# A retention and mixture-of-experts kernel: the retention cut into twelve steps of 64 tokens of both batches, its products in 64 by 64 tiles

## The reference

```python
for t in range(S):                       # retention, per batch and head
    state = gamma[h] * state + outer(k[t], v[t])
    y[t] = q[t] @ state / sqrt(D)        # x = y, heads side by side, 512 wide
logits = x @ w_gate                      # 8 experts
local_gate = sigmoid(x @ w_local)
for each batch, for s in range(S):       # routing: a scan along the tokens
    e = argmax(logits[s]) if s == 0 or local_gate[s] < 0.5 else e_of_token_before
    p = softmax(logits[s])
    out[s] = p[e] * (relu(x[s] @ w1[e]) @ w2[e])
```

## Time and profile before

| | us |
|---|---|
| median of 3 runs | 266.32 (265.81 to 267.69) |
| the profiled execution | 265.87 |
| its span in the trace | 264.1 |
| TensorE's granted clock over the span | 0.993 of full |
| retention loop, first masked product to `x_transpose` | 8.52 to 66.61 |
| first product of the experts (L1085) | 68.74 |

### The profile page before, as it was taken

One profiled execution on the slowest core, in us unless ns is written; L12 is line 12 of the kernel. 1 busy time (PEld: TensorE's weight loads), 2 busy tenths in 40 slices (PEclk: granted clock), 3 DMA queues, 4 the chain that ended last, 5 costly groups with the idle time before them and its releaser, 6 DMA issues.

```text
span 264.1 us, 4970 instructions
## 1 busy us (share of the span) xinstructions
PE 253.7 (96%) x1935; PEld 216.3 (82%) x1935; DVE 196.4 (74%) x408; ACT 135.5 (51%) x253; POOL 60.1 (23%) x57
## 2 busy tenths in 40 slices
PE   8899999998999999999999999999999999999991
PEld 3688887887887888888988888898898889889891
DVE  2445899996996796987789598588859858877700
ACT  1313637457559273485477438457644835753310
POOL 0473333531004331006104201500510240011011
PEclk9999999999999999999999999999999999999997
DMA  5999999942202818187538808925861890620000
GB/s 183 359 414 412 413 412 412 426 182 79 82 1 72 367 64 315 70 318 249 211 130 306 353 2 318 351 96 196 313 273 37 315 380 33 251 104 34 0 37 34
DMA packets 11386, 56.82 MB, mean 215 GB/s; under 512 B 1751, under 2 KB 2135, under 8 KB 9570
## 3 DMA queue, kind: packets, MB, share of 16 engines
q1 hardware_dynamic: 7056, 45.95, 45.2%
q0 software_dynamic: 2560, 7.34, 7.3%
q10 hardware_dynamic: 1746, 3.19, 3.2%
HBM read 50.19 MB, written 7.34 MB: 218 GB/s over the span
## 4 chain that ended last, share of the span: by engine, by line
PE 80%; DVE 12%; ACT 2%; DMA 2%; issue 2%; POOLq 0%; SPq 0%; DVEq 0%
PE ps L1085 21%; PE ps L1087 10%; PE ps L1104 10%; PE ps L1105 10%; PE ps L1106 10%; PE ps L972 3%; PE ps L984 3%; PE ps L1065 2%; DVE scores_masked L754 2%; DVE w_split L767 2%; PE ps L1017 2%; PE ps L1007 2%; PE ps L1128 2%; ACT slot_values L487 2%; DMA qkv_sb<-qkv 2%
## 5 line engine op out<-in xcount | busy, mean ns | idle before, releaser
L1085 PE MATMUL ps<-x_sorted_T,w_split 128*128 128x480 f32 (+1 forms) x288 | 89.4, 370 | 0.2 <-DVE x_sorted_T L780 0.2
L1087 PE MATMUL ps<-x_sorted_T,w_split 128*128 128x240 f32 (+1 forms) x288 | 75.5, 262 | 0.0
L774 DVE TENSOR_TENSOR w_split<-w_raw,w_split 128x1024 fp32r<-128x1024 f32 x56 | 66.1, 1219 | 6.8 <-ACT w_split L493 6.8
L787 DVE TENSOR_REDUCE h_sums<-ps 128x240 f32<-128x480 f32 (+1 forms) x72 | 43.0, 598 | 23.8 <-PE ps L1087 22.8
L1085 PEld LDWEIGHTS ps<-x_sorted_T,w_split 128*128 128x128 f32 x288 | 54.1, 188 | 7.1 <-issue 0.3
L493 ACT CAST w_split<-w_raw 128x1024 fp32r<-128x1024 f32 x56 | 55.8, 1042 | 4.7 <-DMA w_raw<-w 4.7
L1087 PEld LDWEIGHTS ps<-x_sorted_T,w_split 128*128 128x128 f32 x288 | 54.7, 190 | 0.3
L502 ACT ACTIVATE hT<-h_sums 128x240 fp32r<-128x240 f32 (+1 forms) x72 | 27.1, 380 | 52.8 <-DVE h_sums L787 52.8
L1104 PE MATMUL ps<-w_split,hT 128*128 128x512 f32 x120 | 48.3, 402 | 0.0
L386 POOL DMA_INDIRECT out<-y_rows,scatter_idx x16 | 17.1, 1068 | 135.0 <-ACT y_rows L510 130.7
L1105 PE MATMUL ps<-w_split,hT 128*128 128x512 f32 x120 | 47.4, 395 | 0.0
(11 more groups left out here) (130 smaller groups left out, 265.6 us busy)
## 6 DMA issues: line engine op xcount, KB each, us to landing
w_raw<-w SPq DMA_DIRECT2D x14, 2048.0 KB, 9.2
qkv_sb<-qkv SPq DMA_DIRECT2D x22, 512.0 KB, 12.9
w_raw<-w SPq DMA_DIRECT2D x8, 512.0 KB, 15.5
x_rows<-x_rows_sb ACTq DMA_DIRECT2D x12, 256.0 KB, 6.7
qkv_sb<-qkv SPq DMA_DIRECT2D x2, 256.0 KB, 13.2
out<-y_rows,scatter_idx POOLq DMA_INDIRECT x16, 5.0
x_gathered<-x_rows,gather_idx POOLq DMA_INDIRECT x15, 7.8
c_route_sb<-c_route SPq DMA_DIRECT2D x1, 146.0 KB, 9.5
```

Of the source, the lines that this page charges most:

```text
L774: V.tensor_tensor(ws[:, par, 1, half, at:at + PIECE], raw[:, half, at:at + PIECE], ws[:, par, 0, half, at:at + PIECE].bitcast(fp32), ALU.s ...
L787: V.tensor_reduce(hs[:, f % 3, 0:n * ROWS], h_ps[f % 3][:, 0:2 * n * ROWS].rearrange("p (a t) -> p t a", a=2), AX.X, ALU.add).then_inc(h_s ...
L1085: MM(at[:, 0:2 * w].rearrange("p (a t) -> p a t", a=2), ws[:, par, 0, 0, cols], xTs[:, k, :, sub], start=(k == 0), stop=(k == KD - 1), ski ...
L1087: last = MM(at[:, w:2 * w], ws[:, par, 1, 0, cols], xTs[:, k, 0, sub], start=False, stop=(k == KD - 1), skip_group_check=True)
```

## The change

The retention's step is 64 tokens (C = 64) of both batches side by side, 12 steps again. The scores of a step are then 64 by 64 blocks, one for each head and batch, and all four phases have 16 float32 products of 64 by 64 tiles with 64 streamed, in an order in which four that follow each other use four different quarters of the array. PE's phases sum: `from_state` and `state_products` now miss at one step each (the first and the last) instead of at two.

With it:

- masks and `q_decays` are for 64 tokens. `masked` is one instruction of 512 elements a partition, not two.
- the state is kept in SBUF for both batches (512 elements a partition, not 256) and DVE adds a step's products to it (`st + u_ps`). Its decay goes into q: POOL makes `q_now` (`q_scale`, 256 elements a partition, once a step) and multiplies q by it.
- the step's output has one PSUM buffer of two banks, and `from_state` waits for ACT's copy of the step before. `from_chunk` is in two halves around `state_products`.
- the order on PE, ACT and DVE inside a step is new; the routing groups have 2, 3, 3 and 4 steps. A group's scan is two instructions (one for each batch), `to_col` has two products for each step.
- the pieces of expert 0's weights are loaded at other steps, the last three behind all of q, k, v; the router's and w1's rows are reordered on the host to fit the new order of heads.

```diff
+C = S // 12
-NX = NC * B
+NX = S // C
-GC = 3
-GROUPS = NX // GC
+GROUP_AT = (0, 2, 5, 8, NX)
```

The loads on SP:

```diff
+            e0_piece(0)
             for m in range(4, NX):
                 if m >= SLOTS:
                     sp.wait_ge(y_done, m - SLOTS + 1)
                 load_half(m, 0)
                 load_half(m, 1)
-                if m >= 4:
-                    e0_piece(m - 4)
+                if m in (5, 6, 7, 9):
+                    e0_piece({5: 1, 6: 2, 7: 3, 9: 4}[m])
+            for p in range(5, 2 * PIECES):
+                e0_piece(p)
```

POOL:

```diff
+            def q_scale(m):
+                pool.wait_ge(qdec_ready, 1)
+                if m > 1:
+                    pool.wait_ge(q_ready, m - 1)
+                nc.gpsimd.tensor_tensor(q_now[:, :, :], q_dec[:, :, :],
+                                        s_dec[:, m, :].unsqueeze(2).to_broadcast([P, HP, C]),
+                                        ALU.mult).then_inc(q_scaled, 1)
+            for m in range(NX - 1):
+                if m == 0:
+                    k_decayed(0)
+                    q_scale(1)
+                else:
+                    q_scale(m + 1)
+                    k_decayed(m)
+                q_decayed(m + 1)
```

ACT's loop:

```diff
             for m in range(NX):
+                xT_out(m)
+                if m in KEEP_AT:
+                    exps(KEEP_AT[m])
+                    keep_row(KEEP_AT[m])
+                if m in E0_MID:
+                    e0_high(E0_MID[m])
+                if m == GROUP_AT[2] + 3:
+                    slot_values(1, range(2))
+                if m < NX - 1:
+                    logits_out(m)
+                    rows_out(m)
+                if m == GROUP_AT[1] + 3:
+                    slot_values(0, range(size(0)))
+                if m == GROUP_AT[2] + 3:
+                    slot_values(1, range(2, size(1)))
+                for p in E0_END.get(m, ()):
+                    e0_high(p)
```

DVE, its two operations of a step and its loop:

```diff
             def masked(m):
                 dve.wait_ge(qk_done, m + 1)
-                for r in range(2):
-                    V.tensor_tensor(sm[:, m % 2, r, :, :], sc_ps[r], masks[:, r, :, :], ALU.mult).then_inc(m_ready, 1)
+                V.tensor_tensor(sm[:, m % 2, :, :, :].rearrange("p r n t -> p r (n t)"), sc_ps,
+                                masks.rearrange("p r n t -> p r (n t)"), ALU.mult).then_inc(m_ready, 1)
             def state(m):
-                dve.wait_ge(u_done, b * (NC - 1) + c + 1)
-                V.tensor_tensor(st[:, :, :], u_ps, s_dec[:, c + 1, :].unsqueeze(2).to_broadcast([P, HP, D]),
-                                ALU.mult).then_inc(s_ready, 1)
+                dve.wait_ge(u_done, m + 1)
+                dve.wait_ge(qk_done, m + 2)
...
+                    V.tensor_tensor(st[:, :, :, :], st[:, :, :, :], u_ps, ALU.add).then_inc(s_ready, 1)
...
             for m in range(NX):
+                if m in COL_AT:
+                    route_c(COL_AT[m])
+                if m < NX - 1:
+                    state(m)
+                    masked(m + 1)
+                if m in COL_AT:
+                    route_d(COL_AT[m])
+                    if COL_AT[m] < 2:
+                        slot_match(COL_AT[m])
...
+                if m in A_AT:
+                    route_a(A_AT[m])
+                if m in KEEP_AT:
+                    route_b(KEEP_AT[m])
+                if m in E0_LOW:
+                    e0_low(E0_LOW[m])
```

PE, `qk` (the other phases in the same manner) and its loop:

```diff
+                for n in range(HP):
+                    for r in range(2):
+                        for b in range(B):
+                            rows, half = slice(r * D, (r + 1) * D), slice(b * C, (b + 1) * C)
+                            last = MM(sc_ps[half, r, n * C:(n + 1) * C], io[rows, s, 1, n, half],
+                                      io[rows, s, 0, n, half], start=True, stop=True)
...
             for m in range(NX):
+                if m in COL_AT:
+                    to_col(COL_AT[m])
+                if m > 0:
+                    from_state(m)
+                from_chunk(m, 0)
+                if m < NX - 1:
+                    state_products(m)
+                from_chunk(m, 1)
+                if m == NX - 1:
+                    break
+                qk(m + 1)
+                if m in KEEP_AT:
+                    to_rows(KEEP_AT[m])
...
+                rows_and_logits(m)
```

The tables of steps:

```diff
+A_AT = {GROUP_AT[g + 1]: g for g in range(GROUPS - 1)}
+KEEP_AT = {at + 1: g for at, g in A_AT.items()}
+COL_AT = {at + 2: g for at, g in A_AT.items()}
+E0_MID = {6: 2}
+E0_END = {2: (0,), 4: (1,), 7: (3,), 9: (4,), 10: (5, 6)}
+E0_LOW = {3: 0, 5: 1, 6: 2, 8: 3, 9: 4, 10: 5, 11: 6}
```

More of the change, by code:

```diff
@@ L987, in state_products @@
-            def state_products(m):
-                b, c = divmod(m, NC)
-                s = m % SLOTS
-                pe.wait_ge(k_ready, b * (NC - 1) + c + 1)
-                for n in range(HP):
-                    for r in range(2):
-                        rows = slice(r * D, (r + 1) * D)
-                        last = MM(u_ps[rows, n, :], kd[:, m % 2, 2 * n + r, :], io[:, s, 3, n, rows],
-                                  start=(c == 0 and n == 0), stop=True, skip_group_check=True)
-                last.then_inc(u_done, 1)
@@ L999, in from_chunk @@
-            def from_chunk(m):
-                s = m % SLOTS
-                pe.wait_ge(kv_in[s], 16 * (m // SLOTS + 1))
-                pe.wait_ge(m_ready, m * 2 + 2)
-                for n in range(HP):
-                    for r in range(2):
-                        rows = slice(r * D, (r + 1) * D)
-                        last = MM(y_ps[m // (NX - 1)][rows, n, :], io[:, s, 3, n, rows], sm[:, m % 2, r, n, :],
-                                  start=(m % NC == 0 and n == 0), stop=True, skip_group_check=True)
-                last.then_inc(y_done, 1)
+                pe.wait_ge(q_ready, m)
@@ new lines, in from_state @@
+                pe.wait_ge(s_ready, m)
+                pe.wait_ge(xT_ready, m)
+                for pair in range(2):
+                    for b in range(B):
+                        for r in range(2):
+                            for n in range(2 * pair, 2 * pair + 2):
+                                rows = slice(r * D, (r + 1) * D)
+                                MM(y_at(n, r, b), st[rows, b, n, :], qd[rows, m % 2, n, b * C:(b + 1) * C],
+                                   start=(pair + b == 0), stop=False, skip_group_check=True)
@@ new lines, in from_chunk @@
+            def from_chunk(m, other):
+                s = m % SLOTS
+                if other == 0:
+                    pe.wait_ge(kv_in[s], 16 * (m // SLOTS + 1))
+                    pe.wait_ge(m_ready, m + 1)
+                else:
+                    pe.wait_ge(y_half, m + 1)
+                for pair in range(2):
+                    for r in range(2):
+                        for n in range(2 * pair, 2 * pair + 2):
+                            b = r ^ other
+                            half = slice(b * C, (b + 1) * C)
+                            last = MM(y_at(n, r, b), io[half, s, 3, n, r * D:(r + 1) * D], sm[half, m % 2, r, n, :],
+                                      start=(m + pair + other == 0), stop=True, skip_group_check=True)
+                last.then_inc((y_half, y_done)[other], 1)
@@ new lines, in state_products @@
+            def state_products(m):
+                s = m % SLOTS
+                pe.wait_ge(k_ready, m + 1)
+                for n in range(HP):
+                    for b in range(B):
+                        for r in range(2):
+                            rows, half = slice(r * D, (r + 1) * D), slice(b * C, (b + 1) * C)
+                            last = MM(u_ps[rows, b, n, :], kd[half, m % 2, 2 * n + r, :], io[half, s, 3, n, rows],
+                                      start=True, stop=True, skip_group_check=True)
+                last.then_inc(u_done, 1)
@@ L1280, in constants @@
     t = np.arange(P)
+    i = t % C
     def parts(x):
```

447 lines of the change are left out of this document (214 added, 233 removed).

## The result

The changed kernel takes 283.55 us (282.96 to 286.05) beside 267.0 (265.81 to 267.69) of the kernel before in the same rounds: ratio 1.064, 95% interval 1.056 to 1.072. It is slower, where 261.0 was forecast; the range of 255.5 to 270 doesn't hold it. The profiled execution took 283.36 us, its span is 281.2. Ratios are of the faster runs alone: two of e7's ten runs and one of e8's four, slower than the fastest by over 1.5%, count in the medians given but not in the ratios.

The account below looks back on a forecast made before the run. The prediction took PE to bound the loop, with DVE second and loads third. From the profiled 265.87 us it took 6.2 gained in the loop and 1.2 given back behind it: 260.9, stated as 261.0, range 255.5 to 270.

Parts of the forecast that it names:

- PE's sum: Loop: 23.0 us of phases plus rows_and_logits, routing and the rest, 43.7 us, so PE alone would reach the experts at 52.
- B: Rival, loop: PE's records come no quicker than now, phases 0.96 us, 271.9 us in all; chance 0.28.
- case A: Loop: four tiles run together as summed, experts start at 62.5, likeliest 261.0 us, 255.5 to 264; chance 0.60.
- PE's phases, 0.51 us: Loop: 32 records in groups of four each 57 ns take 0.51 us; 45 phases are 23.0 us for 39.0.
- The granted clock: Loop: the forecast would be wrong if this fell under 1.00, since PE has gaps it never had; no size given.
- DVE, POOL: Loop: DVE needs about 44 us, stalls by POOL included, and idles 9; POOL's work rises from 23.4 to 32.3 us.
- rival C: Loop: four tiles run but routing steps go at DVE's pace; experts start at 66.5, 264.9 us; chance 0.12.
- Loads hidden: Loop: step 11's data arrive at 45 us, pieces 5 and 6 at 48 to 50, PE wants them at 52 to 55.
- Behind the loop, 1.2 us: After the loop: the last group's 4 steps for 3 lengthen the chain through slot_values and table products, 1.2 us given back.

Follow-up runs that it names:

- e7: Changed kernel with its four phases reading only the upper bfloat16 halves of their operands, so half the records in those phases: 268.69 us, ratio 1.005.
- e8: Changed kernel with the load of expert 1's first half of weights waiting until the first gather has landed: 283.45 us, ratio to the kernel before 1.067.
- e1: No kernel computation, only 64 by 64 float32 products in four tiles: a block took 3.45 to 4.0 us without transfers, 5.9 to 6.2 beside all loads.
- e9: As e1, but in the two diagonal tiles only: no stop without transfers, a stop after each block, 6.19 us apart, beside all loads.
- e3: Changed kernel without loads of q, k, v for steps 6 to 11, earlier data reused: experts' first product at 77.29 us; whole 381.35 us, not comparable.

## Why the prediction was wrong

The step that failed is PE's sum, 45 × 0.51 and the 43.7 us built on it: it let PE stand only for data of other engines and put the supply of its instructions at nothing. In its place the runs show PE held up for blocks of instructions, ten stops and 18.1 us in all, and a low clock behind them. The rival that could have caught this, B, was mispriced, and with it the chance of case A. B was named ("records reach it at a pace that fits 110 ns pairs but not four each 57 ns"), with the two paces, 72 records in 4.7 us and 136 in 3.5; but it was priced as a slower phase, 45 × 0.96, so that 271.9 was its end. The phases were never slower than forecast at the full clock. The supply is a budget over many phases: 48 ns a record beside all loads (e1 and e9), 29 in the mean without (e1). The kernel before asks for one each 66 ns, the forecast for one each 26. From the trace of before that budget couldn't be measured, but its lower side, 66 ns, was there, and 45 × 32 + 11 × 8 = 1528 records at 66 would have been 101 us, where B had 43.2 + 13.6: the upper end of the range was no bound at all.

By the forecast's own steps:

- **PE's phases, 0.51 us**: right (0.51, groups of four each 57 ns). The rule of the Trainium skill set against it, "TensorE: Matmul & The Clock Gate", section "Back-to-back issue gap", about 25 ns from one matmul's start to the next at 64 columns and fewer, doesn't hold across tiles: 32 records in 0.51 us are 16 ns each.
- **PE's sum, 43.7 us, the experts not held by PE**: wrong. PE was busy for 52.2 us, stood in ten stops for 18.1 and waited otherwise for 4.5, where the forecast had 10.8 of waits (54.5 less 43.7): 8.5 + 18.1 - 6.3, with a start 0.4 later, are the 20.7 us between 62.5 and 83.15. The Trainium skill has the mechanism in "Runtime: NRT & Kernel Launch", section "Instruction fetch mechanics": blocks of 16 KiB, 256 instructions, fetched by the sequencer over a DMA queue of its own. The counts of 126 and 128 records agree, and so do the queue's packets, one before each resumption. Its word that the cost is mostly hidden does not: a stop took 1.8 us in the mean here, and 5.0 once. The forecast hadn't weighed that page of the Trainium skill.
- **The granted clock**: the last part called the forecast wrong with a clock under 1.00, and it was 0.50 to 0.84 from 20 to 45 us. It fell after the long stops, and made phases and `rows_and_logits` up to twice as long. No price for this stood in the sum; the 8.5 us that PE was busy beyond the forecast fit it, but no run separates them.
- **DVE, POOL**: the sizes were right (`masked` 683 ns × 12, `state` 686 for 0.68, `q_scale` 612 for 0.6) but for `k_decayed`, 1.32 us for 1.05, so that POOL was busy 35.3 us for 32.3. DVE was busy 40.5 us of 44, but idle for 32 instead of 9: it stood behind PE.
- **What was left once supply is no limit**: e7's start at 67.72 is 5.2 us later than A's 62.5 and 1.2 later than rival C's 66.5, with DVE at 98% in the routing steps as C had it. Of the 20.7 us between forecast and result, 15.4 go in e7 (83.15 to 67.72) with the records and the shorter phases together, and 5.2 stay, with waits for DVE and ACT, two stops and the low clock. How they divide is open.
- **Loads hidden**: right for the data, for which PE never stood in the loop; but the same loads made the instructions late: a block lasted 6.2 instead of 3.7 us. I had looked at what the loads carry, not at what they slow.
- **Behind the loop, 1.2 us**: 2.7. The wait for `slot_row_onehot` grew by 0.7; the rest is a low clock in the experts' first products. From 83.15 to the first row below three pairs take 1.33 us, where a pair takes 0.22 at the full clock, and from 95.05 to 98.66 the nine `down` products take 0.40 us each in the mean for 0.23 before, 1.5 in all. The forecast's own term, the chain through `slot_values`, is not on the path that ended last any more: this term failed in its mechanism too.

```profile
84.48 0.39 PE L1158 MATMUL ps<-x_sorted_T,w_split 128*128 128x240 f32 x1
```

Shown: that PE's stops come with blocks of instructions, in two tiles as in four, and lengthen with loads (e1, e9, e3); that the stops go, but for two, when the records are halved (e7). Not shown: where a block's packet waits before it starts, behind other packets on the DMA engines or elsewhere; it is no plain function of the bytes moved, since the longest interval, 8.3 us (44.87 to 53.19), came at 258 GB/s (42 to 53 us), where 6.1 to 6.4 came at some 410. Nor is the low clock's share of the loss. Not tried: a version with four tiles and few records, as `from_state` with 128 streamed in tiles of heads, which would need another layout of the output.

## What to carry to other kernels

Count PE's records per microsecond before cutting products into small tiles: here the tiles halved a phase's time and doubled its instructions. Here one record each 66 ns was free, one each 52 too, and 48 ns beside full loads (29 without) was the mean floor, however fast the tiles run; one block came only at 66 ns a record. A stop named issue every 126 to 128 records with nothing waited for is its mark; and what an engine loses in such a stop comes back as a lower clock behind it.

## What the runs showed of the hardware that was not expected

- A block of PE's instructions (126 to 128 float32 records) arrives each 3.45 to 4.0 us with idle DMA, each 5.9 to 6.4 us beside loads at some 410 GB/s; 213 (changed kernel) to 351 records (e1) ran before the first stop.
- PE resumed 2.3 to 2.5 us after the block's packet had started (changed kernel); the packet takes some 1 us, with loads or without, and starts 1.1 to 1.5 us after the last resumption with idle DMA, 3.6 to 4.0 beside full loads (e1, changed kernel).
- A small float32 record has a price of its own that depends on the tiles: 53.5 ns on the whole array with 16 columns streamed, 62 with 64-row, 128-column weights and 64 streamed (1.98 us for 32), 37 in pairs of tiles with 32 streamed, 14 to 16 in four tiles of 64 by 64 with 64 streamed.
- The granted clock was 0.50, its lower level of 1.2 GHz, from 20 to 25 us, behind a stop of 2.48 us; it had not been under 1.00 in this stretch before.
